# Layer 2 of a two-layer network by seven half-size block products, with its combined weights made during layer 1

## The reference

```python
def phi(x):                       # x already scaled by 64**-0.25
    h = einsum('bhsd,md->bhsm', x, omega) - sum(x * x, -1) / 2
    return exp(h - max(h, -1)) / sqrt(128)
kv, z = einsum('bhsm,bhsd->bhmd', phi(k), v), sum(phi(k), 2)
x = einsum('bhsm,bhmd->bhsd', phi(q), kv) / (einsum('bhsm,bhm->bhs', phi(q), z) + 1e-6)
x = x.transpose(0, 2, 1, 3).reshape(2304, 512)
h = x @ w_in;  x = (h * clip(h + 3, 0, 6) / 6) @ w_out            # layer 1
h = x @ w_in2; x = (h / (1 + exp(-1.702 * h))) @ w_out2           # layer 2
```

## Time and profile before

| | |
|---|---|
| runs, us | 916.42, 918.49, 917.99; median 917.99 |
| span of the profiled execution, us | 914.6 |
| own time of the profiled execution | not recorded apart from its span; median less span is 3.4 us |
| PE busy | 909.7 us, 99% |
| DVE, ACT, POOL busy | 431.8, 380.8, 171.3 us |
| DMA | 53.01 MB, mean 58 GB/s |

### The profile page before, as it was taken

How to read it: one execution, slowest core, us unless ns; L and a number is a source line. 1 busy time by engine, 2 the same in 40 slices (tenths; PEclk the granted TensorE clock), 3 DMA queues, 4 the chain that set the end, 5 groups by cost and what they waited for, 6 DMA issues and landing times.

```text
span 914.6 us, 12760 instructions
## 1 busy us (share of the span) xinstructions
PE 909.7 (99%) x4843; PEld 766.0 (84%) x4843; DVE 431.8 (47%) x802; ACT 380.8 (42%) x869; POOL 171.3 (19%) x184
## 2 busy tenths in 40 slices
PE   8999999999999999999999999999999999999998
PEld 8988888888888888888889888888888888888897
DVE  6976777756677666632233632242223223322332
ACT  6857655554455544522236722232223222222323
POOL 2765564220222200000018700000000000000000
DMA  8635652443224432200006310010001000100000
GB/s 275 193 104 139 152 132 68 91 91 61 55 68 91 91 57 34 71 1 0 1 12 175 114 23 2 1 46 1 1 1 47 0 1 1 47 1 0 13 35 24
DMA packets 102349, 53.01 MB, mean 58 GB/s; under 512 B 83216, under 2 KB 83856, under 8 KB 102288
## 3 DMA queue, kind: packets, MB, share of 16 engines
q1 hardware_dynamic: 80864, 49.54, 20.4%
q10 hardware_dynamic: 21424, 2.65, 2.0%
HBM read 40.44 MB, written 4.72 MB: 49 GB/s over the span
## 4 chain that ended last, share of the span: by engine, by line
PE 98%; DVE 1%; DMA 0%; ACT 0%; issue 0%; DVEq 0%
PE acc L803 13%; PE acc L811 13%; PE acc L810 13%; PE hid L743 11%; PE hid L719 11%; PE hid L744 11%; PE att L743 4%; PE att L744 4%; PE att L719 4%; PE att L658 3%; PE att L621 3%; PE acc L756 2%; PE acc L757 2%; PE acc L758 1%; PE acc L621 1%; PE att L607 1%
## 5 line engine op out<-in xcount | busy, mean ns | idle before, releaser
L803 PE MATMUL acc<-g_hi,w_out_hi 128*128 128x512 f32 x512 | 200.4, 391 | 0.0
L811 PE MATMUL acc<-g_hi,w_out_lo 128*128 128x512 f32 x508 | 197.8, 389 | 0.0
L810 PE MATMUL acc<-g_lo,w_out_hi 128*128 128x512 f32 x508 | 197.7, 389 | 0.0
L743 PE MATMUL hid<-x_hi,w_in_hi 128*128 128x512 f32 (+1 forms) x476 | 177.9, 374 | 0.1
L744 PE MATMUL hid<-x_hi,w_in_lo 128*128 128x512 f32 (+1 forms) x476 | 175.2, 368 | 0.0
L719 PE MATMUL hid<-x_lo,w_in_hi 128*128 128x512 f32 (+1 forms) x476 | 175.0, 369 | 0.0
L1279 DVE TENSOR_TENSOR g_lo<-R,g_hi 128x512 fp32r<-128x512 f32 (+1 forms) x159 | 107.7, 677 | 86.7 <-ACT g_hi L978 86.5
L978 ACT ACTIVATE g_hi<-R 128x512 fp32r<-128x512 f32 (+1 forms) x159 | 93.9, 590 | 84.7 <-DVE R L1274 52.6
L811 PEld LDWEIGHTS acc<-g_hi,w_out_lo 128*128 128x128 f32 x508 | 95.3, 188 | 20.2
L803 PEld LDWEIGHTS acc<-g_hi,w_out_hi 128*128 128x128 f32 x512 | 96.2, 188 | 19.1
L810 PEld LDWEIGHTS acc<-g_lo,w_out_hi 128*128 128x128 f32 x508 | 95.4, 188 | 18.8
(11 more groups left out here) (200 smaller groups left out, 1189.9 us busy)
## 6 DMA issues: line engine op xcount, KB each, us to landing
X<-w_in SPq DMA_DIRECT2D x16, 256.0 KB, 3.1
X<-w_out SPq DMA_DIRECT2D x16, 256.0 KB, 3.4
out_t<-X SPq DMA_DIRECT2D x16, 256.0 KB, 2.2
rows<-q_n SPq DMA_DIRECT2D x14, 288.0 KB, 3.2
rows<-k_n SPq DMA_DIRECT2D x14, 288.0 KB, 3.4
q_phi<-q_blocks SPq DMA_DIRECT2D x106, 36.0 KB, 2.1
v_rows<-v_n SPq DMA_DIRECT2D x14, 256.0 KB, 3.5
q_cols<-q_t SPq DMA_DIRECT2D x11, 256.0 KB, 2.9
```

The source lines that it names most:

```text
L743: nc.tensor.matmul(bank, w_hi[0][:, at], x_hi[:, k, x0:x0 + t], start=(k == 0), stop=False)
L803: nc.tensor.matmul(bank, w_hi[1][:, at], g_hi[:, g, 0:t], start=(s == 0), stop=False)
L810: nc.tensor.matmul(bank, w_hi[1][:, at], g_lo[:, g, 0:t], start=False, stop=False)
L811: last = nc.tensor.matmul(bank, w_lo[1][:, at], g_hi[:, g, 0:t], start=False, stop=(s == J - 1))
```

## The change

Layer 2 no longer works in chunks and steps. The tokens are cut in three blocks of 768 (`SUPERS`), and each of the two matrix products of a block is done as a 2x2 block product with seven half-size products (`PRODUCTS`) in place of eight. One unit is one half-size product of one group of 256 by 256 weights with 384 tokens: 12 matmuls of 384 columns. A block has 28 units for the hidden part (4 groups of 7) and 28 for the output part (7 products by 4 groups), so layer 2 has 168 units. The sums in PSUM are taken out between units in a fixed order (`keep_first`, `take`), and the sums of activations that the scheme needs are made on GpSimd (`x_first_sums`, `third_and_second_sums`, `fourth_sum` and others).

In the diff `load_raw`, `store_combos` and `load_combos` are SyncE's, `prepare` is GpSimd's, `combined` TensorE's (one unit), `high_combos` ScalarE's (called last in a step's turn) and `take` VectorE's.

Of each weight matrix seven combinations are needed, each in a high and a low part. They are made in layer 1 in 32 pieces u (`prepare`, `high_combos`), at the steps given by `prep_step`: pieces 0 to 9 at steps 14, 16, ..., 32, the rest at steps 49 to 63 and at 64, 66, ..., 76. SyncE loads a raw piece (256 KB), and stores its combinations to device memory in four DMAs. Pieces 0 to 9 share one staging buffer, the others have three. In layer 2 SyncE loads each unit's weights (512 KB) into a ring of ten slots. The input is `w_raw2`, in an order made on the host. The last 256 tokens of layer 2 are no longer computed by token.

```diff
+RING = 10
+HALF2 = 384
+EARLY_PREP = 10
+PRODUCTS = ("11", "22", "12", "33", "31", "24", "43")
+CHAIN = {"11": "a", "12": "a", "22": "d", "33": "d", "24": "d", "31": "c", "43": "c"}
+        def prep_step(u):
+            if u < EARLY_PREP:
+                return 14 + 2 * u
+            v = u - EARLY_PREP
+            return 49 + v if v < 15 else 64 + 2 * (v - 15)
+        def load_step(u):
+            return prep_step(u) - (1 if u < EARLY_PREP else 2)
+            def load_raw(u):
...
+                if uses_of(u) > 1:
+                    sp.wait_ge(stored_prep[s], 64 * (uses_of(u) - 1))
+                sp.dma_start(stage(u)[0], w_raw2[u]).then_inc(load_prep[s], 16)
+            def store_combos(u):
...
+                sp.wait_ge(prep_high, 2 * u + 2)
+                sp.dma_start(combos_at(u, slice(0, 3), False), ...)
+                sp.dma_start(combos_at(u, slice(3, 7), False), ...)
+                sp.wait_ge(prep_low, 2 * u + 2)
+                sp.dma_start(combos_at(u, slice(0, 3), True), ...)
+                sp.dma_start(combos_at(u, slice(3, 7), True), ...)
+            def load_combos(i):
...
+                    sp.wait_ge(unit_done, i - RING + 1)
...
+                sp.dma_start(ring[slot], combos[kind, q, FACTOR[PRODUCTS[p]]]).then_inc(load_unit[slot], 16)
+            for g in range(2 * L2):
...
+                if g % 2 == 0:
+                    for u in preps_at(g // 2 - 1, prep_step):
+                        store_combos(u)
+                    for u in preps_at(g // 2, load_step):
+                        load_raw(u)
+            def prepare(u):
...
+                pool.wait_ge(load_prep[stage_of(u)], 16 * uses_of(u))
+                nc.gpsimd.tensor_tensor(s1, third, fourth, ALU.add).then_inc(prep_added, 1)
...
+            def combined(i, moving):
...
+                pe.wait_ge(load_unit[i % RING], 16 * (i // RING + 1))
+                for m in range(2):
+                    to = sums(CHAIN[name])[:, m, :]
+                    for k in range(2):
+                        nc.tensor.matmul(to, w[:, at:at + P], high[:, k, :], ...)
+                        nc.tensor.matmul(to, w[:, at + P:at + 2 * P], high[:, k, :], ...)
+                        last = nc.tensor.matmul(to, w[:, at:at + P], low[:, k, :], ...)
+            def high_combos(u):
+                raw, sums_u, high, sums_high = stage(u)
+                act.wait_ge(load_prep[stage_of(u)], 16 * uses_of(u))
+                nc.scalar.activation(high, raw[:, 0:3 * P], ACT.Copy).then_inc(prep_high, 1)
+                act.wait_ge(prep_added, 4 * u + 4)
+                nc.scalar.activation(sums_high, sums_u, ACT.Copy).then_inc(prep_high, 1)
...
+                for u in preps_at(n, prep_step):
+                    high_combos(u)
+                if n - LAST1 - 12 in (0, 1):
+                    x_high(0, n - LAST1 - 12)
+            def take(g, what, part, i):
+                dve.wait_ge(unit_done, i + 1)
...
+                    nc.vector.tensor_tensor(part(what), sums("c"), part(what), ALU.add).then_inc(taken, 1)
```

More of the change, by code:

```diff
@@ new lines, in build @@
+        xc_frees = (10, 10, 16, 16, 16, 16, 16)
+        xc = [[at_place(f"x{part}_{name}", [P, 2, HALF2], xc_places[i], F32R) for part, i in zip(("hi", "lo"), both)]
+              for name, both in zip(PRODUCTS, xc_order)]
+        x_sum_rows = at_place("x_sum", [P, KC, CH_MAX], parts_base + KC * BLOCK)
+        R2 = at_place("gate2", [P, 2, 2, HALF2], gates_base + PART)
+        g2 = [at_place(f"g2_{i}", [P, 2, 2, HALF2], rows_base + 2 * i * PART, F32R) for i in range(GROUPS2)]
+        late = [at_place(f"stage{i}", [P, 1920], stage_base + i * 1920 * 4) for i in range(3)]
@@ new lines, in preps_at, with stage_of, uses_of, stage @@
+        def preps_at(n, step):
+            return [u for u in range(PREPS) if step(u) == n]
+        def stage_of(u):
+            return 3 if u < EARLY_PREP else (u - EARLY_PREP) % 3
+        def uses_of(u):
+            return u + 1 if u < EARLY_PREP else (u - EARLY_PREP) // 3 + 1
+        def stage(u):
+            if u < EARLY_PREP:
+                raw, sums, high, sums_high = (x_at(k, TOKENS - S, 512) for k in range(KC))
+            else:
+                x = late[stage_of(u)]
+                raw, sums, high, sums_high = x[:, 0:512], x[:, 512:1024], x[:, 1024:1408], x[:, 1408:1920]
+            return raw, sums, high[:, 0:3 * P].bitcast(F32R), sums_high.bitcast(F32R)
@@ L768, in ends @@
[L768 to L774, removed]
-                for half in range(2):
-                    for n in steps:
-                        last = row_products(n, acc[2 + half], 1, half * WIDE // 2, WIDE // 2, n == steps[0], n == steps[1])
-                    last.then_inc(acc_done, 1)
+                row_products(n, acc[1], 1, 0, WIDE, s == 0, s == J - 1).then_inc(out_done, 1)
@@ L850, in _ @@
             hidden(0, (3,))
-            for n in range(2 * L2):
-                if 0 < n < 2 * L2 - 1:
+            for n in range(L2):
+                if 0 < n:
                     hidden(n)
-                if n == 2 * L2 - 2:
-                    hidden(n + 1)
                 if n == 2:
@@ L870, in _ @@
                     attend(a, what)
-            ends()
+            for c in range(SUPERS):
+                for q in range(GROUPS2):
+                    for p in range(len(PRODUCTS)):
+                        if (c, q, p) == (0, 0, 2):
+                            output(L2 - 1)
+                        hidden_product(c, q, p)
+                for p in range(len(PRODUCTS)):
+                    output_product(c, p)
         @block.scalar
```

596 lines of the change are left out of this document (466 added, 130 removed).

## The result

The changed kernel takes 974.35 us (median of 4 runs, 973.57 to 974.66); before takes 917.35 (4 runs, 916.42 to 918.49). The ratio is 1.0622 with a 95% interval of 1.0607 to 1.0637: slower, as forecast, by 57.0 us where 28.9 were forecast. Each run stands 1.8 us above its own span (973.57 and 971.8; 916.42 and 914.6).

The account below looks back on a forecast made before the run. TensorE's stream was taken as the bound, PE being busy 99% of the span. -45.2 + 41 + 4.2 + 15.0 + 12.6 + 1.3 = +28.9 on a span of 914.6, so 947 us for the runs, range 935 to 960.

Parts of the forecast that it names:

- stream of layer 2: TensorE in layer 2: 2016 matmuls of 384 columns at 0.1727 us each, 348.2 us in all, 45.2 less.
- five waits in layer 1: Layer 1, pieces 1, 3, 5, 7, 9: raw loads queue behind a crossing's moves, gates come late; 41 us.
- clock behind them: TensorE at half clock after each of five layer 1 pauses, 2.1 us each, 10.5 in all.
- layer 1 to 2: Steps 76 and 77: GpSimd's sums of x and 768-column high and low parts delay the gates; 4.2 us.
- row moves ahead of unit 10: Layer 2 start: unit 10's load stands behind 32 row moves in SyncE's queue, so TensorE waits 15.0 us.
- clock behind that wait: TensorE at half clock after the pause at unit 10, 2.1 us.
- end: Behind the last matmul: a take of 768 columns and one store of 384 KB, 1.3 us more.
- the wide one: The range for the time that should hold 8 in 10: 912 to 975 us.
- rival 4: Layer 2's hidden groups: GpSimd and VectorE disturb each other, TensorE waits 0.75 us in each of 12; +9, 956 us; chance 0.10.
- Early pieces: Pieces 0 to 9 in layer 1: the odd ones delay gates by 8.5 to 9.1 us each, 41 us charged in all.
- Even pieces: Even-numbered pieces among 0 to 9 in layer 1: loads issued a step earlier without moves, charged nothing.

Follow-up runs that it names:

- all_five: Changed kernel with five edits: early stores and loads before moves, GpSimd's pieces before squares, row moves spread, next-block sums apart, block 0's first sums earlier; 898.00 us.
- prep_first: Changed kernel with the former piece's four stores and the next raw load ahead of a crossing's moves in SyncE's queue; 929.06 us.
- xsums0_split: Changed kernel with GpSimd's two first sums of x for block 0 moved apart, to steps 67 and 71; 970.55 us.
- rows_spread: Changed kernel with the 32 row moves put two behind each ring load from unit 14 on, not ahead of unit 10's load; 957.87 us.
- kept_warm: Changed kernel with 30 extra unused matmuls of 512 columns ahead of each of the five numerators that wait in layer 1; 969.32 us.

## Why the prediction was right, and where its size was off

From the starts of PE, the 57.2 us are: layer 1 to the gate of step 63 +61.9, from there to the gate of step 79 +6.8, layer 2 -12.9, end +1.3 (57.1). By its own steps:

| step of the prediction | forecast | measured |
|---|---|---|
| stream of layer 2 | -45.2 | -43.6 |
| five waits in layer 1 | +41 | +42.3 |
| clock behind them | +10.5 | +12.8 |
| other waits and lateness in layer 1 | 0 | +6.8 |
| layer 1 to 2 | +4.2 | +6.8 |
| row moves ahead of unit 10 | +15.0 | +13.8 |
| clock behind that wait | +2.1 | +2.7 |
| unit 7, for ScalarE (1.32 us), and short waits before unit 10 | 0 | +2.1 |
| output phases, waits and clock | 0 | +12.1 |
| end | +1.3 | +1.3 |

The time lies outside the forecast's own range of 935 to 960 and 0.65 us inside the wide one. That is luck in part: 975 was added up from the upper bounds of the pauses and rival 4, but the pauses came near their middle, and what filled the range were terms put at nothing. Of the forecast's 947 us, 1.6 come from the 3.4 that it put between span and runs, where a run stands 1.8 above its own span.

- **Stream.** 2016 matmuls in 349.7 us, once waits and slow matmuls are taken off (the changed kernel and all_five agree to 0.1): 0.1735 each, where the middle of 256 and 512 columns gave 0.1727. The interpolation of the earlier trace rows was sound.
- **Early pieces.** The place, the chain of waits and the cost held. Each is slightly longer than its sum: four stores behind the moves and not three, and 3.0 us of landing where 2.1 were entered, near the 2.2 of an output store of that size. The gates of steps 17, 21, 25, 29 and 33 come 8.6 to 10.7 us late, 49.7 in sum against 43.8. Their removal (prep_first) gives 45.3 and not the 55 of waits and clock, because the even pieces then show.
- **Even pieces.** "I charge them nothing; their cover is some 5 us of SyncE's idle time" looked at the wrong queue. SyncE was in time; GpSimd had a pair's rows ahead of the piece, and ScalarE waited for it 4.9 us and more. In the changed kernel TensorE pays little for it, as the odd places cost more and come next; they show once these are mended, 3.5 to 9 us.
- **Layer 1 to 2.** The engines that are late are those of the forecast; the size was 2.6 us short, of which 1.7 is the clock behind the wait of 2.7 us. That the first sums make the lateness is shown for 1.7 us at most (xsums0_split); the rest is argued.
- **Row moves.** Right in place and time, shown by rows_spread.
- **Clock.** The earlier trace rows gave 2.1 us for a pause; the six cost 15.5 in sum (12.8 + 2.7), 2.6 each. kept_warm shows that it is a cost of idleness apart from the waits. What the prediction missed is that waits of only 2.7 us, two in the output phases and one on the way to layer 2, cost some 1.7 us of clock each.
- **Rival 4.** The mechanism was the right one, and was placed in the wrong phase: "TensorE waits 0.75 in each of 12 groups". In the hidden groups VectorE's takes have an operand in PSUM and stay at 0.96 us beside GpSimd (the two rows below, POOL and DVE of the changed kernel at one time), and the low part ahead of a take took 1.34 and 1.35 us at 644.5 and 659.1, 0.4 more, well within the 1.15 us in hand; no wait of that kind came. It came in the output phases, where low parts with both operands in SBUF follow one another every 2.07 us and GpSimd has nine instructions in a row; it cost 12.1 us, not 9: 5.7 of the two waits, some 3.3 of clock behind them and 3.2 of shorter waits ahead of them. By the Trainium skill, "GPSIMD Engine Reference", specifications, VectorE's instructions that contend with GpSimd for SBUF are those with two SBUF inputs and those in a two-port mode. The trace agrees for the first kind: 2.0 to 2.6 against 0.94 us, and no change for instructions with an operand in PSUM.

```profile
662.24 1.84 POOL L827 TENSOR_TENSOR G<-G,gate 128x768 f32<-128x768 f32 x1 [2.65 <-ACT gate L1376]
```

```profile
662.36 0.96 DVE L1703 TENSOR_TENSOR G<-acc,G 128x768 f32<-128x768 f32 x1 [1.07 <-PE acc L1065]
```

So the step that failed is the sum's last assumption, that after unit 10 nothing in layer 2 waits, together with the zero for the even pieces and small waits of layer 1: 12.1 + 6.8 of the 28 us that were missing. The direction came from the two waits behind moves in SyncE's queue, and these were right: 42.3 us against 41, and 13.8 against 15.0.

## What to carry to other kernels

Time a new chain by the queue that it stands in, on every engine it passes: here much the same work cost 76 us more or less by its place behind moves, squares and row moves that it does not depend on. Work put beside a full TensorE is free only while each of the others has its next result in time; count the longest row of back-to-back instructions that share a path, not their mean share of busy time. A wait costs more than its length where the clock falls with it.

## What was not expected of the hardware

- A rest of 2.7 us lowered the clock: matmuls of 384 columns ran 0.32 us apart and not 0.17 for about 3 us behind it. It does not do so each time: in kept_warm the clock fell with a rest of 1.93 us and stayed at 1.00 with one of 2.65 (at 573.7). In all_five, waits of up to 1.65 us left the mean granted clock at 1.000.
- A low part of 768 columns with both operands in SBUF takes 0.94 us alone and 2.0 to 2.6 beside GpSimd; GpSimd's sum goes from 1.85 to 2.5. Both lose, VectorE the more.
- Stores to device memory in pieces of 512 bytes take 3.0 to 3.3 us to land for 192 to 256 KB; ring loads of 512 KB take 4.4 (the DMA queues move 252 GB/s from 830 to 960 us and 274 from 720 to 780, beside the full stream).
